# Experts with stationary weights and outputs kept on chip by sorted token, rows stored by an indirect DMA

## The reference

```python
e_idx = np.argmax(x @ w_gate, axis=1)
gate_w = probs[np.arange(N), e_idx]                # softmax of the logits
eom = 1.0 / (1.0 + np.exp(-(x @ w_output_gate)))
for e in range(E):
    mask = e_idx == e
    h = np.maximum(x[mask] @ w1[e], 0.0)
    out[mask] = gate_w[mask, None] * eom[mask, e, None] * (h @ w2[e])
# feed-forward
h = x @ w_in
g = np.maximum(0.01 * h, h)
return g @ w_out
```

## Time and profile before

| | us |
|---|---|
| median of 3 runs (lowest, highest) | 1135.42 (1133.69, 1135.95) |
| profiled execution, its time | 1135.07 |
| profiled execution, its span | 1133.3 |
| TensorE busy, matmuls / weight loads | 967.5 / 849.7 |
| VectorE, ScalarE, POOL busy | 430.1, 438.7, 494.1 |
| relu or copy of 128x512 on ScalarE (L1203, L1208) | 0.60 |
| trailing part of 128x512 on VectorE (L1232) | 0.69 |
| one x_b from issue to landing | 2.5 |

### The profile page before, as it was taken

The page is one execution under the profiler, slowest core; times in us unless marked ns, Lnnn a source line. Parts: engine busy times, 40 slices in busy tenths (PEclk is TensorE's granted clock), DMA queues, the critical chain, the costliest instruction groups (busy, mean ns, idle before and its releaser), DMA issues. The chain is left out here.

```text
span 1133.3 us, 17921 instructions
## 1 busy us (share of the span) xinstructions
PE 967.5 (85%) x5874; PEld 849.7 (75%) x5875; DVE 430.1 (38%) x670; ACT 438.7 (39%) x660; POOL 494.1 (44%) x339
## 2 busy tenths in 40 slices
PE   0249888989997019999999998799999999999998
PEld 0037776777786018999989987699999999999998
DVE  3467767767763602333332322222221222222111
ACT  6767767766531202222222211233333333333322
POOL 0244443444331573743577397424324343343322
PEclk9999888889999559999999999799999999999999
DMA  5223233223220734323434252100001010010000
GB/s 210 72 72 115 59 119 114 78 82 86 76 78 2 271 132 146 113 99 135 153 104 146 93 206 97 57 1 23 34 0 56 0 56 0 0 56 0 29 1 28
DMA packets 48679, 90.56 MB, mean 80 GB/s; under 512 B 23144, under 2 KB 39680, under 8 KB 45056
## 3 DMA queue, kind: packets, MB, share of 16 engines
q1 hardware_dynamic: 43264, 55.46, 15.1%
q0 software_dynamic: 5376, 34.61, 8.8%
HBM read 65.99 MB, written 24.02 MB: 79 GB/s over the span
## 5 line engine op out<-in xcount | busy, mean ns | idle before, releaser
L1397 POOL TENSOR_TENSOR act_r<-act_f,act_r 128x512 fp32r<-128x512 f32 x96 | 124.7, 1299 | 258.1 <-ACT act_r L1442 258.1
L1520 PE MATMUL bank<-x,w_in_r 128*128 (+1 forms) x864 | 219.4, 399 | 1.2 <-DVE x L1475 1.2
L1533 PE MATMUL bank<-w_out_r,act_r 128*128 128x384 f32 x1152 | 217.4, 337 | 0.0
L1533 PEld LDWEIGHTS bank<-w_out_r,act_r 128*128 128x128 f32 x1152 | 204.8, 188 | 8.2
L1520 PEld LDWEIGHTS bank<-x,w_in_r 128*128 128x128 f32 x864 | 161.6, 190 | 31.6 <-DVE x L1475 1.6
L1481 DVE TENSOR_TENSOR act_f<-bank,small 128x512 f32<-128x512 f32 x96 | 66.5, 692 | 284.1 <-ACT small L1439 277.1
L1274 PE MATMUL bank<-wm,x_tr 128*128 x522 | 128.4, 400 | 3.9 <-POOL wm L1178 1.6
L1439 ACT ACTIVATE small<-bank 128x512 f32<-128x512 f32 x96 | 57.5, 599 | 188.3 <-PE bank L1520 186.1
L1296 PE MATMUL bank<-wm,h_tr 128*128 x696 | 128.6, 339 | 1.6 <-DVE h_tr L1232 1.6
L1296 PEld LDWEIGHTS bank<-wm,h_tr 128*128 128x128 f32 x696 | 120.1, 188 | 1.9 <-issue 1.9
L1274 PEld LDWEIGHTS bank<-wm,x_tr 128*128 128x128 f32 x522 | 96.8, 190 | 24.8 <-issue 5.0
(11 more groups left out here) (171 smaller groups left out, 1408.4 us busy)
## 6 DMA issues: line engine op xcount, KB each, us to landing
stage<-moe_w POOLq DMA_DIRECT2D x12, 1536.0 KB, 6.9
qkv_in<-in_qkv SPq DMA_DIRECT2D x24, 576.0 KB, 5.7
a_in<-in_a SPq DMA_DIRECT2D x8, 1152.0 KB, 6.0
x_sorted<-zeros SPq DMA_DIRECT2D x8, 816.0 KB
stage<-moe_w SPq DMA_DIRECT2D x4, 1536.0 KB, 8.1
x_b<-x_sorted SPq DMA_DIRECT2D x31, 192.0 KB, 2.5
y_sorted<-y_b SPq DMA_DIRECT2D x29, 192.0 KB, 1.9
out<-o_sb SPq DMA_DIRECT2D x24, 192.0 KB, 1.9
```

What stands on the lines that cost most here:

```text
L1397: pool.tensor_tensor(a[:, 1, :], act_f[f % 2][:, :], a[:, 0, :].bitcast(F32), ALU.subtract).then_inc(s_gl, 1)
L1520: last = pe.matmul(h_bank[f % 2][:, :], w_in_r[:, wp, t * F2 + f * P:t * F2 + (f + 1) * P], x2[:, xp, bass.ds((w % 2) * (KT * XW) + t * XW ...
L1533: last = pe.matmul(o_bank[j][:, 0:W], a[:, ap, j * P:(j + 1) * P], w_out_r[:, wp, f * W:(f + 1) * W], start=(f == 0 and n == 0), stop=(f = ...
```

## The change

x_sorted is packed: the experts' parts follow each other without padding, and a block may start at any row (its row stands in the table). Each row of it is two words longer (XR = 386) and carries the gate and the token's number; so the gate is worked out ahead of the positions. The clears of x_sorted and y_sorted go, but for two rows per partition at its end. y_sorted is gone. The first weights are staged in quarters instead of halves.

In the experts both layers have the weights stationary, 128 columns at a time, and stream 128 tokens. The hidden rows come out transposed, so neither they nor the result are transposed again. VectorE multiplies x_b by the gate before its transposes. ScalarE applies the relu and writes the leading part in one step, VectorE the trailing part in one step. ScalarE copies the result to y_t, which holds all tokens, transposed, in sorted order in SBUF. The rows beyond an expert's last token are overwritten by the next block. TensorE has one loop for each expert with fixed weight addresses.

The feed-forward is in the same block of the program and reads its tokens from y_t, in sorted order; the gathers, gates and transposes go. The six windows are written out. POOL stores the rows by an indirect DMA after its trailing parts; the numbers of the tokens are read once into ids.

```diff
-    xs = nc.dram_tensor("x_sorted", (TB * P, W), F32, kind="Internal").ap()
-    ys = nc.dram_tensor("y_sorted", (TB * P, W), F32, kind="Internal").ap()
+    xs = nc.dram_tensor("x_sorted", (N + 2 * P, XR), F32, kind="Internal").ap()
...
-                if unit(i, 2):
-
-                    lot = TB * P // UNITS
-                    clear(xs[bass.ds((i - 2) * lot, lot), :], LOT_P, lot // LOT_P)
...
+        @block.sync
+        def _(sp):
+            def load(g):
+                row = at(sp, T_ROW, g, 0, N)
+                sp.dma_start(x_b[:, :], xs[bass.ds(row, P), :]).then_inc(s_xb, 16)
+
+            load(0)
+            sp.dma_start(ids[:, :].unsqueeze(2),
+                         xs[0:N, W + 1:W + 2].bitcast(I32).rearrange("(t p) a -> p t a", p=P),
+                         allow_slow_non_contiguous=True).then_inc(s_ids, 16)
...
+            def scatter(w):
                 for j in range(TW):
...
+                    pool.wait_ge(s_o, TW * (w + 1) + j + 1)
+                    pool.indirect_dma_start(
+                        out=out, out_offset=bass.IndirectOffsetOnAxis(ap=ids[:, TW * w + j:TW * w + j + 1].bitcast(U32), axis=0),
+                        in_=o_sb[j][:, :], in_offset=None).then_inc(s_out[j], 16)
...
             def body(w, more):
+                for f in range(2, FT2):
+                    trail(w, f)
                 if more:
...
+                    for f in range(2):
+                        trail(w + 1, f)
+                scatter(w)
...
+            def leading(g):
+                for j in range(2):
+                    act.wait_ge(s_p1, 2 * g + j + 1)
+                    act.activation(h_tr[:, 0, j * 512:(j + 1) * 512], hid_bank[j][:, :], ACT.Relu).then_inc(s_hh, 1)
+
+            def result(g):
+                col = at(act, T_ROW, g, 0, N)
+                act.wait_ge(s_p2, g + 1)
+                act.activation(y_t[:, :, bass.ds(col, P)], ye_bank[:, 0:W].rearrange("p (k t) -> p k t", k=KT),
+                               ACT.Copy).then_inc(s_y, 1)
...
+            with act.Fori(0, last_g) as g:
+                leading(g)
+                result(g)
+
+            act.wait_ge(s_wq, 4 * E + 4)
+            act.wait_ge(s_y, last_g + 1)
             for j in range(TW):
...
                 tokens(0, j)
+            leading(last_g)
+            result(last_g)
...
+            with dve.Fori(0, last_g) as g:
+                gated(g + 1)
+                trailing(g)
+                block_tokens(g + 1)
...
+            def layer1(e, g):
+                w1 = wm[:, e % 2, :, :]
...
+                for j in range(2):
+                    pe.wait_ge(s_hl, 2 * g + j + 1)
+                    for i in range(HF):
+                        f = j * HF + i
+                        for n, (xp, wp) in enumerate(((0, 0), (0, 2), (1, 0))):
+                            for t in range(KT):
+                                last = pe.matmul(hid_bank[j][:, i * P:(i + 1) * P],
+                                                 w1[:, wp, t * F1 + f * P:t * F1 + (f + 1) * P],
+                                                 x_tr[:, xp, t * P:(t + 1) * P],
+                                                 start=(t == 0 and n == 0), stop=(t == KT - 1 and n == 2))
+                    last.then_inc(s_p1, 1)
+
+            def layer2(e, g):
...
+                for j in range(2):
+                    for part, pairs in enumerate((((0, 1), (0, 3)), ((1, 1),))):
+                        pe.wait_ge(s_hl if part else s_hh, 2 * g + j + (3 if part else 1))
+                        for i in range(HF):
+                            f = j * HF + i
+                            for hp, wp in pairs:
+                                for d in range(KT):
+                                    last = pe.matmul(ye_bank[:, d * P:(d + 1) * P],
+                                                     w2[:, wp, f * W + d * P:f * W + (d + 1) * P],
+                                                     h_tr[:, hp, f * P:(f + 1) * P],
...
+            for e in range(E):
+                with pe.Fori(ends[e - 1] if e else 0, ends[e]) as g:
+                    layer1(e, g)
+                    transpose_block(g + 1)
+                    layer2(e, g)
```

More of the change, by code:

```diff
@@ L139, in attention @@
     PR = HL + D
-    x_t = stage[:, 0:HP * C]
-    flip1, whole, cosv, sinv = [stage[:, 2 * W + j * GW:2 * W + (j + 1) * GW] for j in range(4)]
+    x_t = sb(ctx, "x_t", [P, HP * C])
+    flip1, whole, cosv, sinv = [sb(ctx, n, [P, GW])[:, :] for n in ("flip1", "whole", "cosv", "sinv")]
     flip = [flip0[:, :], flip1]
@@ L1101, in _ @@
         def _(sp):
[L1102 to L1115 removed]
+            sp.wait_ge(s_zeros, 1)
@@ new lines, in _, with experts_then_feed_forward, late @@
+            sp.dma_start(xs[N:N + 2 * P, :].rearrange("(p r) w -> p r w", p=P),
+                         zeros[:, :].unsqueeze(1).to_broadcast([P, 2, XR])).then_inc(s_fill, 16)
+            for u in range(6):
+                if u >= 2:
+                    sp.wait_ge(s_split, u - 1)
+                sp.dma_start(stage[:, u % 2 * QE:(u % 2 + 1) * QE],
+                             moe_w[u // 4][:, u % 4 * QE:(u % 4 + 1) * QE]).then_inc(s_stage[u % 2], 16)
+            sp.wait_ge(s_fill, 16)
+def experts_then_feed_forward(nc, ctx, sem, sb, bank, ident, ids, table, stage, stage_at, masks_at, wm, wbase, w_out_r, y_t,
+                              moe_w, w_in, w_out, xs, out, s_stage, s_w):
+    T_ROW, T_CUM, T_LAST = 0, TB, TB + E
+    WE = KT * F1
+    QE = WE // 2
+    HF = FT1 // 2
+    XW = TW * P
+    w_in_r = nc.alloc_sbuf_tensor_at("w_in_r", [P, 2, KT * F2], F32R, offset=wbase)
+    place = [wbase + 4 * 4 * WE]
+    def late(name, shape, dt=F32):
+        t = nc.alloc_sbuf_tensor_at(name, shape, dt, offset=place[0])
+        place[0] += (4 * math.prod(shape[1:]) + 31) // 32 * 32
+        return t
+    x_b = nc.alloc_sbuf_tensor_at("x_b", [P, XR], F32, offset=masks_at)
@@ L1374, in _, with split @@
         @block.gpsimd
         def _(pool):
-            def gather(w, after):
-                if after:
-                    pool.wait_ge(s_tx, TW * w)
-                pool.tensor_tensor(idx[:, :], pos[:, bass.ds(TW * w, TW)], zero[:, :], ALU.add).then_inc(s_idx, 1)
-                pool.wait_ge(s_idx, w + 1)
-                pool.tensor_tensor(spare[:, :], zero[:, :], zero[:, :], ALU.add)
+            lots = [moe_w[e] for e in range(E)] + [w_out, w_in]
+            def split(lot, q, lead, trail, done):
+                u = 4 * lot + q
+                part = stage[:, u % 2 * QE:(u % 2 + 1) * QE]
+                if u < 6:
+                    pool.wait_ge(s_stage[u % 2], 48)
+                else:
+                    pool.wait_ge(s_more[u % 2], 16 * ((u - 6) // 2 + 1))
+                if q == 0 and done is not None:
+                    pool.wait_ge(s_p2, done)
+                pool.tensor_scalar(lead, part, 1.0, 0.0, ALU.mult, ALU.add).then_inc(s_ws, 1)
+                pool.wait_ge(s_ws, u - 3)
+                pool.tensor_tensor(trail, part, lead.bitcast(F32), ALU.subtract).then_inc(s_wq, 1)
+                pool.wait_ge(s_wq, u - 3)
+                if u + 2 < 4 * len(lots):
+                    nxt = lots[(u + 2) // 4]
+                    pool.dma_start(part, nxt[:, (u + 2) % 4 * QE:((u + 2) % 4 + 1) * QE]).then_inc(s_more[u % 2], 16)
@@ new lines, in quarter @@
+            def quarter(pair, q):
+                return pair.rearrange("p a n -> p (a n)")[:, q * QE:(q + 1) * QE]
+            for e in range(1, E):
+                done = at(pool, T_CUM, e - 2, 1, NBMAX) if e >= 2 else None
+                for q in range(4):
+                    split(e, q, quarter(wm[:, e % 2, 0:2, :], q), quarter(wm[:, e % 2, 2:4, :], q), done)
+            for q in range(4):
+                split(E, q, w_out_r[:, 0, q * QE:(q + 1) * QE], w_out_r[:, 1, q * QE:(q + 1) * QE], None)
```

521 lines of the change are left out of this document (183 added, 338 removed).

## The result

The changed kernel takes 1750.05 us (median of 4 runs, 1749.43 to 1753.34), the kernel before 1134.7 (4 runs, 1133.69 to 1135.95): a ratio of 1.543, 95% interval 1.540 to 1.546. Slower, as forecast, but by 615 us and not by 173. The profiled execution has a span of 1748.5 us and a mean granted clock of 0.707, where the kernel before had 0.947.

A forecast was written before the change was run, and what follows sets the result against it. Experts and feed-forward were taken as bound by TensorE's matmuls, other stages by their chains; -2 + 2.2 + 192 - 12.8 - 2.9 - 6.4 + 3 = +173.1 on 1135.1, plus 0.35, gave 1308.5 us; range 1288 to 1366.

The forecast's parts named there:

- The failed step: Start of the expert stage: the slow clock adds about 2.5 us, within 5 us added for the start.
- that term: Expert stage: 4176 load-and-matmul pairs 111 ns apart, blocks of 16.3 us, stage 478 against 286.1 us, +192 us.
- Rival C: Expert matmuls: a narrow fp32r matmul runs like full fp32, 222 ns, total 1772 us; chance 0.06.
- Rival A: Expert matmuls: columns are the bound, loads hide, distance 66 ns, total 1120 us, faster; chance 0.09.
- B: Expert matmuls: loads in between, about 89 ns a pair, total 1217 us; chance 0.05.
- Change-over: Between experts and feed-forward: only the result copy and hand-overs remain, 0.8 us instead of 13.6, -12.8 us.
- The -2.9 for the clock: First 27 wide matmuls of the feed-forward: no gap for the clock to fall in, -2.9 us.
- Feed-forward: 20 transposed tiles in the windows go, 0.32 us each, -6.4 us; POOL's scatters stay hidden.
- End: After the last matmul: indirect scatters replace plain stores, issued 1.3 us apart and landing 2.1 us after issue, +3 us.
- Routing: Before the experts: scatters start 1.5 us later, gate multiply before the first transpose +0.7, together +2.2 us.
- Attention: Clears of 816 KB go from SP's queue: -2 us, between 0 and -10.

The follow-up runs named there:

- e_free: Changed kernel with 16 wide matmuls between TensorE's register loads before the first transposes and 4 behind them, in idle time: 1316.04 us.
- e_warm: Changed kernel with 48 matmuls of 512 columns, into a bank nobody reads, ahead of the first expert block: 1328.73 us.
- e_n64: Changed kernel with each expert matmul streaming 64 columns instead of 128: 1755.05 us.
- e_m64w: e_warm with every expert matmul loading 64 of the 128 stationary columns, still streaming 128: 1132.89 us.
- e_plain: e_free with the feed-forward's output stored by plain DMAs on SP's queue instead of POOL's indirect DMAs: 1309.24 us.
- the first eight experiments: Edits of the changed kernel in streamed columns, wide matmuls, a stop or loaded columns: 1355.96, 1755.05, 1328.73, 1950.39, 1552.19, 1551.23, 1316.04, 1132.89 us.
- g256b: Changed kernel rewritten for groups of 256 tokens, warmed as in e_free, last group's relus ahead of the wait for feed-forward weights: 1123.9 us, ratio 0.987 to the kernel before.

## Why the prediction was wrong

**The failed step** is in the start of the expert stage: "about 2.5 for the slow clock (the first 18 matmuls took 5.72 instead of 4.38 us)". It took for granted that the new stream pulls the clock up as the old one did. The old one had 512 columns to a load in those 18 matmuls, the new one 128, and that one stays where it was, at 1.2 GHz: 909 us at 0.50. The slow clock was put at 2.5 us and cost 909.4 - 477.1 = 432 us, the stage of e_free being the one at full clock. No rival had the clock in it, and no term of the range; beside attention and routing the range held the distance of pairs at full clock alone, from 108 to 125 ns. The row that should have raised the question was used: the earlier trace rows shows how a gap drops the clock. What the earlier trace rows shows, pairs at 111 ns, it shows at a granted clock of 1, and the prediction said so and did not ask what the clock would be at the new place.

**The rest of that term was right.** The distance at full clock is 112 ns (e_warm), forecast 111; the load is its cause (e_n64, e_m64w); 4176 pairs; the stage 477.1 us (e_free), forecast 478; TensorE without waits. Entered at full clock the changed kernel takes 1316 us, within the range of 1288 to 1366. (By its own terms the upper end was 1308.5 + 58 + 5 = 1371; the 5 us of attention and routing were left out of it. Nothing hangs on that.)

**Rival C** priced 222 ns a pair and 1772 us, 22 us from what came, by luck. Its reason is false: a narrow fp32r matmul is no slower kind of matmul; the same instruction takes 112 ns in e_warm. A near number for a wrong reason would have led to the wrong remedy, to give up the layout where 20 matmuls in idle time were wanted. Rival A's 66 ns and B's 89 were not seen with a load of 128 columns.

**Change-over**: forecast -12.8, measured -12.9. The -2.9 for the clock did not come in the changed kernel: the stage ended at half clock, and the first 27 wide matmuls took 8.67 us. In e_free, which ends it at full clock, the 27 take their 6.4.

**Feed-forward**: forecast -6.4 - 2.9 = -9.3; -7.6 in the changed kernel, and from 901.72 to 1303.31 = 401.6, so -9.9, in e_free. The transposes cost what was said, and POOL's scatters delay nothing, as worked out.

**End**: forecast +3, measured 1748.5 - 1737.56 = 10.9 against 2.9, so +8.0. The last scatters stand where they were expected:

```profile
1731.12 6.43 PE L1453 MATMUL bank<-w_out_r,act_r 128*128 128x384 f32 x36
...
1736.79 0.99 POOL L1241 DMA_INDIRECT out<-o_sb,ids  x1 [2.12 <-ACT o_sb L1288]
...
1740.63 0.97 POOL L1241 DMA_INDIRECT out<-o_sb,ids  x1 [0.31 <-issue]
```

The last one's issue ends at 1741.60 and it lands some 2.6 us later, but the program ends at 1748.5: some 4 us more, in which no record stands. A stretch that may be of the same kind was to be seen in the trace of before, between the last scatter of routing and POOL's next instruction:

```profile
410.63 0.96 POOL L1006 DMA_INDIRECT x_sorted<-x_all,pos  x1 [0.30 <-issue]
415.74 2.75 POOL L1174 TENSOR_SCALAR wm<-stage 128x3072 fp32r<-128x3072 f32 x1 [4.15 <-POOLq L992]
```

It is 4.15 us, and the prediction counted 2.1 for the landing of a scatter. That the scatters make the end longer is shown (e_plain); what POOL does in that time is not, nor that the two stretches are the same thing.

**Routing**: forecast +2.2, measured +2.5, in other shares. The columns as in the timelines above:

```profile
413.00 0.97 POOL L997 DMA_INDIRECT x_sorted<-x_all,pos  x1 [0.30 <-issue]
...
419.77 3.42 POOL L1213 TENSOR_TENSOR wm<-stage,wm 128x1536 fp32r<-128x1536 f32 x1
421.88 1.52 DVE L1335 TENSOR_SCALAR x_b<-x_b 128x384 f32<-128x384 f32 x1 [24.08 <-DMA x_b<-x_sorted]
```

From the first step behind attention to the last scatter's end it took 49.4 us (364.58 to 413.97) where it took 48.9, so +0.5 and not +1.5; from there to the first transposes 9.7 where it was 7.6, so +2.0 and not +0.7. The first gate multiply is 1.52 us long beside POOL's subtraction; the median of the 30 is 0.42. With the hand-over behind it (to 423.64) it accounts for 1.8 of the 2.0 us.

**Attention**: the forecast -2 can't be read. That step comes at 364.58 us, 362.71 before, but nine kernels with the same attention (this one and the first eight experiments) have it between 363.3 and 370.9. A change of 2 us there is below what one trace of each can tell.

## What to carry to other kernels

The distance of matmuls is a property of the instructions and of the clock at which they run. Whenever a change makes a stream narrower, ask apart from its speed at full clock whether that stream will bring TensorE to full clock, and whether it will get back there after the next gap; where the trace has no such stream that rises by itself, half speed belongs among the rivals. Where a stage of narrow matmuls must stand, put some wide ones into the idle time just ahead of it and behind every stop, and where the weight load is the bound, give each load more columns: 256 cost 120 ns where 128 cost 112, and that stream raised the clock by itself.

## What the runs showed of the hardware that was not expected

- A stream of load-and-matmul pairs in fp32r with 128 columns loaded and 128 streamed holds either level of the clock. Entered at half clock it ran 909 us at 213 ns a pair without rising; entered at full clock it ran 477 us at 112 ns without falling. Pairs that stream 64 columns, and the mixture with 16 wide matmuls in a block of 144 narrow ones, stayed at half too; pairs that stream 256 columns rose in the first block, and so did pairs that load 64 and stream 128 (e_m64w, behind its stop). Which property of a stream decides was not isolated further: the earlier trace rows are narrow fp32 matmuls in attention at full clock, and the runs don't show what brought them there.
- The Trainium skill, "TensorE: Matmul & The Clock Gate", section "What's actually happening", says that activity releases the throttle; by the profile's busy time, 908.05 of 909.38 us, this stream was active, and it was not released. The measurement decides.
- A pair bound by its load takes 213 ns at half clock and 112 at full clock, 1.9 times: the load goes by TensorE's clock too. Its own record lasts 333 ns on average in the changed kernel and 192 in e_warm.
- The end of a program behind indirect stores is 8 us longer than behind plain ones (11.0 and 2.9 us). In g256b it is 13.9 us (from 1110.1 to 1124.0), though its last four scatters are issued at the same pace (the last at 3.1 us behind the last matmul's end); why it is longer there stays open.
- VectorE's gate multiply takes 0.42 us, but four of the 30 in the changed kernel took 1.27 to 3.57 us, each beside a split of weights on POOL (L1211, L1213).
